# One wait for each TensorE instruction, and new places of the attention items' steps, in a fused attention and two-layer feed-forward kernel

## The chip, the cores and the metric

One NeuronCore of a Trainium2 chip runs the whole program. The metric is the device time of one execution in microseconds, the median of three runs. The engines are called TensorE (PE, with PEld for its weight loads), VectorE (DVE), ScalarE (ACT), GpSimd (POOL) and SyncE (SP).

## The reference

```python
# attention: q, k, v are (4, 8, 576, 64)
scores = scale * np.matmul(q, k.transpose(0, 1, 3, 2))
mask = block_i >= block_j                       # blocks of 64 positions
scores = np.where(mask, scores, -1000000000.0)
scores = scores - np.max(scores, axis=-1, keepdims=True)
attn = np.exp(scores)
attn = attn / (np.sum(attn, axis=-1, keepdims=True) + 1e-09)
out = np.matmul(attn, v)                        # -> x, (2304, 512)
# first layer
h = x @ w_in                                    # (2304, 2048)
g = np.where(h >= 1, h, np.where(h <= -1, 0.0, (h + 1) ** 2 / 4))
x = g @ w_out                                   # (2304, 512)
# second layer
h = x @ w_in2
g = h * np.cos(h)
return g @ w_out2
```

## The kernel before

**Precision.** Each operand of a product is split into a rounded part (`_hi`) and a remainder (`_lo`). A product of two is made of three matmuls (hi by hi, hi by lo, lo by hi), or of two where the two halves are stacked. So nearly every tensor is made twice: a copy on ScalarE (`x_hi`, `k_hi`, `q_hi`, `v_hi`, `pt_hi`, `g_hi`, `win_hi`, `wout_hi`), and a subtraction on VectorE (`x_lo`, `q_lo`, `pt_lo`, `win_lo`) or GpSimd (`k_lo`, `v_lo`, `g_lo`, `wout_lo`).

**Items.** Attention is cut into 64 items. The first 32, the early ones, are a head's first 256 queries (two tiles of 128), and the last 32, the late ones, are a head's other 320 queries (tiles of 128, 128 and 64). An item goes through these steps: scores on TensorE (`score`, L984), the row maximum on VectorE, the exponential with its row sums on ScalarE, the inverse of the sums on VectorE, the normalisation on GpSimd (`norm`), the transposes on TensorE (`turn`, L1008, into PSUM banks `turned` or `heads_out`), their split (`pt_hi` on ScalarE, `pt_lo` on VectorE), the weighing of V on TensorE (`weigh`, L1024, into `heads_out`), the move of one half of the result on ScalarE, and its addition on VectorE, which writes the feed-forward layer's input. The first and the third tile's transposes of a late item share the bank `turned`: the third tile's (`turn(n, 2)`) wait until `pt_lo` has read the first's.

**Stages.** Nine items run alone (0 to about 65 us), two beside each other in their own banks. The other 55 run beside the first layer's first seven tiles of 256 tokens (to about 540 us). Then come the first layer's last two tiles and the second layer's nine (from about 645 us), eight of them in a loop that the hardware runs. A tile of a layer is eight pairs of hidden blocks: `make_hidden` (L1076) fills a PSUM bank, the other engines activate it, and `use_hidden` (L1095) multiplies the result into `acc`, two pairs later. After a tile ScalarE reads `acc` out (`y_stage`, L696) and splits the next tile's input (`split_next_x`, L689).

**What sets the order.** Every engine runs its instructions in the order in which its own block of the program issues them. The items' steps are spread over slots: an item takes 11 slots (early) or 19 (late), and the table `AT` says at which slot of the item each step is issued, one number for each of three kinds of item: alone, early beside the layer, late. All engines walk the same slots, and within one slot the order of the `if`s in their `attention` function decides. Beside the layer `slots_beside` puts about two slots beside each half of a unit; a half is six matmuls of `make_hidden` or `use_hidden`. A late item so lasts about 10.5 us. `SPLIT_AT` and `LOAD_AFTER` say at which place the first layer's weight pieces are split (`win` on ScalarE and VectorE, `wout` on ScalarE and GpSimd) and after which item they are loaded.

**Waits.** Every step waits for counting semaphores of the steps it needs. On TensorE several waits stand directly ahead of one matmul, for instance ahead of both score matmuls:

```python
pe.wait_ge(q_lo_made, n + 1)
pe.wait_ge(k_lo_made, n + 1)
if late(n):
    pe.wait_ge(exp_made, first_tile(n) + (2 if i == 4 else 0))
```

Of the kernel before, what the change touches and what calls it, by code (L numbers as in the profile page):

```python
# [22 lines left out]
KC = DM // P  # L23
# [3 lines left out]
LAG = 2  # L27
# [42 lines left out]
def stat(n, i):  # L70
# [11 lines left out]
    "score": (0, 0, 0), "score_c": (0, 0, 7), "turn": (14, 12, 11), "turn_b": (0, 0, 16),  # L82
    "turn_c": (0, 0, 19), "weigh": (18, 18, 21), "k_hi": (-9, -9, -10), "q_hi": (-9, -8, -11),
    "v_hi": (8, 9, 6), "exp": (6, 3, 0), "exp_b": (6, 3, 2), "exp_c": (0, 0, 8),
    "pt_hi": (14, 11, 10), "pt_hi_b": (0, 0, 12), "pt_hi_c": (0, 0, 15), "move": (19, 16, 21),
    "q_lo": (-6, -7, -8), "max": (1, 0, 0), "max_b": (1, 0, 2), "max_c": (0, 0, 7),
    "inv": (5, 4, 2), "inv_b": (6, 4, 6), "inv_c": (0, 0, 11), "pt_lo": (14, 12, 15),
    "pt_lo_b": (0, 0, 17), "pt_lo_c": (0, 0, 19), "add": (19, 18, 23), "k_lo": (-9, -10, -11),
    "norm": (3, 3, 3), "norm_b": (6, 3, 5), "norm_c": (0, 0, 8), "x_hi": (20, 0, 0),
    "x_lo": (21, -3, -8), "begin": (20, -3, -6), "v_lo": (14, 7, 6),  # L90
# [20 lines left out]
def user_before(n):  # L111

    return n - 2 if n < ALONE else n - 1

# [30 lines left out]
SPLIT_AT = ((1, 3, 5, 9, 12, 17, 20, 24), (7, 10, 16, 18, 22, 26, 30, 35))  # L145
LOAD_AFTER = ((-1, 1, 4, 7, 9, 11, 12, 14), (-1, 8, 10, 12, 13, 15, 16, 17))
# [32 lines left out]
def attention_feed_forward(nc, qk_early, qk_late, v_early, v_late, w1_in, w1_out, w2_in, w2_out, x2_dram, out):  # L179
    with ExitStack() as ctx:  # L180
# [801 lines left out]
        def _(pe):  # L982
            def score(n, i):
                e = i - tiles_of(n)[0]  # L984
                pe.wait_ge(q_lo_made, n + 1)
                pe.wait_ge(k_lo_made, n + 1)

                if late(n):
                    pe.wait_ge(exp_made, first_tile(n) + (2 if i == 4 else 0))
                elif n > ALONE:  # L990
                    pe.wait_ge(exp_made, first_tile(n - 1) + e + 1)
                elif n > 1:
                    pe.wait_ge(exp_made, first_tile(n - 1 if n < ALONE else n))
# [6 lines left out]
                for into, first, end in pieces:  # L1000
                    nc.tensor.matmul(into, q_tile, k_hi_of(n)[:, first:end], start=True, stop=False)  # L1001
                    last = nc.tensor.matmul(into, q_tile, k_lo_of(n)[:, first:end], start=False, stop=True)  # L1002
                last.then_inc(scores_made, 1)

            def turn(n, e):
# [8 lines left out]
                elif user_before(n) >= 0:  # L1014
                    pe.wait_ge(pt_lo_made, first_turn(user_before(n) + 1))
# [177 lines left out]
```

## Time and profile before

| | |
|---|---|
| median of 3 runs | 1045.59 us (1045.02 to 1050.85) |
| the profiled execution | 1051.79 us |
| its span, first to last instruction | 1049.6 us |
| mean granted TensorE clock over the span | 0.981 |
| busy: TensorE, its weight loads | 1001.9 us (95%), 943.1 us (90%) |
| busy: VectorE, ScalarE, GpSimd | 657.0 (63%), 590.8 (56%), 426.5 us (41%) |
| matmuls | 7360 |

The profile is of one execution, and its durations belong to that one. A matmul's duration is modelled and overlaps the next one's, so how fast TensorE goes is read from the distances between starts, and short waits do not show as idle time of PE. Its weight load precedes each matmul; a wait that a matmul carries holds this load.

### The profile page before, as it was taken

How to read it: one execution, taken by the hardware profiler on the slowest of the kernel's cores; microseconds unless marked ns; L12 is line 12 of the kernel's file. 1: busy time of each engine (PE TensorE's matmuls, PEld its weight loads, DVE VectorE, ACT ScalarE, POOL GpSimd, SP SyncE). 2: the span in 40 equal slices, each digit the busy share in tenths (PEclk: the TensorE clock that was granted, in tenths of full speed). 3: DMA queues.
4: the chain of work that ended last, by engine and by line, in shares of the span. 5: the costliest groups of instructions: out<-in, count | busy, mean ns of one | idle time of the engine just before them, and what ended most of it. 6: DMA issues, size and time to landing. Idle time of an engine off the chain costs nothing.

```text
span 1049.6 us, 19879 instructions
## 1 busy us (share of the span) xinstructions
PE 1001.9 (95%) x7360; PEld 943.1 (90%) x7360; DVE 657.0 (63%) x1422; ACT 590.8 (56%) x1232; POOL 426.5 (41%) x446
## 2 busy tenths in 40 slices
PE   4688999999999999999999999999999999999997
PEld 3578999999999999999999998999999999999995
DVE  5567777766766767666732378656565555656553
ACT  5567776766666666666633356544444444445442
POOL 3559765555555554655522221222222222222211
PEclk9579999999999999999999999999999999999999
DMA  4335321221211212121200144010110101001000
GB/s 133 104 118 157 98 90 65 72 70 49 92 49 53 89 49 72 70 72 65 69 31 22 41 161 162 1 40 0 40 40 0 40 0 40 21 19 40 0 21 21
DMA packets 30886, 62.28 MB, mean 59 GB/s; under 512 B 3680, under 2 KB 11872, under 8 KB 30816
## 3 DMA queue, kind: packets, MB, share of 16 engines
q1 hardware_dynamic: 29664, 57.16, 17.1%
q10 hardware_dynamic: 1152, 4.19, 1.1%
q8 instruction: 43, 0.70, 0.3%
q14 instruction: 27, 0.22, 0.1%
HBM read 51.90 MB, written 9.44 MB: 58 GB/s over the span
## 4 chain that ended last, share of the span: by engine, by line
PE 79%; DVE 9%; ACT 5%; issue 3%; POOL 1%; DMA 1%; ACTq 0%; POOLq 0%; DVEq 0%
PE hidden L1090 33%; PE acc L1107 18%; PE acc L1115 12%; PE heads_out L1036 4%; PE scores L1001 4%; PE turned L1019 3%; PE scores L1002 3%; DVE neg_max L800 1%; PE heads_out L1019 1%; DVE x_lo L879 1%; PE hidden L1073 1%; DVE wout_lo L865 1%; DVE work L885 1%; ACT probs L616 1%; DVE pt_lo L817 1%
## 5 line engine op out<-in xcount | busy, mean ns | idle before, releaser
L543 POOL TENSOR_TENSOR g_lo<-work,g_hi 128x512 fp32r<-128x512 f32 x144 | 187.9, 1305 | 450.7 <-ACT g_hi L713 450.7
L1090 PE MATMUL hidden<-x_hi,win_hi 128*128 128x256 f32 x1136 | 323.5, 285 | 2.8 <-DVE work L912 1.2
L1090 PE MATMUL hidden<-x_hi,win_lo 128*128 128x256 f32 x1136 | 317.9, 280 | 0.0
L1090 PE MATMUL hidden<-x_lo,win_hi 128*128 128x256 f32 x1136 | 317.9, 280 | 0.0
L1090 PEld LDWEIGHTS hidden<-x_hi,win_hi 128*128 128x128 f32 x1136 | 214.3, 189 | 7.6 <-issue 2.0
L1090 PEld LDWEIGHTS hidden<-x_lo,win_hi 128*128 128x128 f32 x1136 | 214.2, 189 | 3.3
L1090 PEld LDWEIGHTS hidden<-x_hi,win_lo 128*128 128x128 f32 x1136 | 216.4, 190 | 0.0
L1115 PE MATMUL acc<-g_hi,wout_hi 128*128 128x256 f32 x576 | 167.4, 291 | 0.3 <-ACT y_stage L696 0.3
L1115 PE MATMUL acc<-g_lo,wout_hi 128*128 128x256 f32 x576 | 160.6, 279 | 0.0
L1115 PE MATMUL acc<-g_hi,wout_lo 128*128 128x256 f32 x576 | 160.5, 279 | 0.0
L513 POOL TENSOR_SCALAR probs<-probs,row_inv 64x576 f32<-64x576 f32 (+2 forms) x160 | 107.4, 675 | 121.6 <-DVE row_inv L812 120.8
L723 ACT ACTIVATE work<-work 128x512 f32<-128x512 f32 x72 | 45.5, 632 | 140.3 <-DVE work L902 140.3
L616 ACT ACTIVATE probs<-scores,neg_max 64x576 f32<-64x576 f32 (+2 forms) x160 | 90.5, 567 | 58.6 <-DVE neg_max L800 56.5
L1107 PE MATMUL acc<-wout_hi,g_hi 128*128 128x512 f32 x288 | 113.7, 395 | 1.6 <-POOL g_lo L543 1.6
L1107 PE MATMUL acc<-wout_hi,g_lo 128*128 128x512 f32 x288 | 113.4, 394 | 0.0
L1107 PE MATMUL acc<-wout_lo,g_hi 128*128 128x512 f32 x288 | 112.6, 391 | 0.0
L1115 PEld LDWEIGHTS acc<-g_hi,wout_hi 128*128 128x128 f32 x576 | 108.9, 189 | 1.2 <-issue 0.4
L1115 PEld LDWEIGHTS acc<-g_lo,wout_hi 128*128 128x128 f32 x576 | 109.2, 190 | 0.6
L912 DVE TENSOR_TENSOR work<-hidden,work 128x512 f32<-128x512 f32 x72 | 49.8, 692 | 94.9 <-ACT work L725 94.9
L1115 PEld LDWEIGHTS acc<-g_hi,wout_lo 128*128 128x128 f32 x576 | 108.9, 189 | 0.0
L713 ACT ACTIVATE g_hi<-work 128x512 fp32r<-128x512 f32 x144 | 89.8, 624 | 14.7 <-DVE work L890 12.3
L800 DVE TENSOR_REDUCE neg_max<-scores 64x1 f32<-64x576 f32 (+2 forms) x160 | 86.8, 543 | 17.7 <-PE scores L1002 13.1
(91 smaller groups left out, 1830.1 us busy)
## 6 DMA issues: line engine op xcount, KB each, us to landing
qk_raw<-qk_late SPq DMA_DIRECT2D x32, 448.0 KB, 3.2
qk_raw<-qk_early SPq DMA_DIRECT2D x32, 256.0 KB, 2.6
v_raw<-v_late SPq DMA_DIRECT2D x32, 160.0 KB, 3.3
x_raw<-x_scratch SPq DMA_DIRECT2D x9, 512.0 KB, 3.5
out<-y_stage SPq DMA_DIRECT2D x36, 128.0 KB, 2.4
x_raw<-w_in SPq DMA_DIRECT2D x8, 512.0 KB, 3.6
y_stage<-w_out SPq DMA_DIRECT2D x8, 512.0 KB, 3.5
x_scratch<-y_stage ACTq DMA_DIRECT2D x8, 512.0 KB, 2.7
```

The costliest lines, as they stand in the source:

```text
L513: nc.gpsimd.tensor_scalar(tile, tile, row_inv[0:rows_of(i), col:col + 1], 1.0, ALU.mult, ALU.mult).then_inc(probs_made, 1)
L543: nc.gpsimd.tensor_tensor(g_lo[:, m % G_RING, :], work[:, m % 2, :], g_hi[:, m % G_RING, :], ALU.subtract).then_inc(g_lo_made, 1)
L616: nc.scalar.activation(tile, scores_tile(n, i), ACT.Exp, bias=neg_max[0:rows_of(i), col:col + 1], accum_out=row_sum[0:rows_of(i), col:col ...
L713: nc.scalar.activation(g_hi[:, m % G_RING, :], work[:, m % 2, :], ACT.Copy).then_inc(g_hi_made, 1)
L723: nc.scalar.activation(work[:, m % 2, :], work[:, m % 2, :], ACT.Abs).then_inc(angle_abs, 1)
L800: nc.vector.tensor_reduce(out=neg_max[0:rows_of(i), col:col + 1], in_=scores_tile(n, i), axis=AX_XY if i == 4 else AX_X, op=ALU.max, negat ...
L912: nc.vector.tensor_tensor(work[:, m % 2, :], hidden[:, m % 2, :], work[:, m % 2, :], ALU.mult).then_inc(hidden_read, 1)
L1001: nc.tensor.matmul(into, q_tile, k_hi_of(n)[:, first:end], start=True, stop=False)
L1019: last = nc.tensor.transpose(turned_of(n, e)[:, at:at + q], probs_chunk(n, i, j), ident[0:q, 0:q])
L1090: last = nc.tensor.matmul(into, w[:, p, c, half * P:(half + 1) * P], x[:, c, :], start=(i == 0), stop=(i == len(products) - 1))
L1107: last = nc.tensor.matmul(acc[:, a, :], g[:, slot, at:at + P], w[:, p, half, :], start=(p == 0 and half == 0 and i == 0), stop=(end and i ...
L1115: last = nc.tensor.matmul(into, w[:, p, half, d * P:(d + 1) * P], g[:, slot, half * TOK:(half + 1) * TOK], start=(p == 0 and half == 0 and ...
```

## The change

It does three things. TensorE's waits are spread so that almost every instruction carries one: a wait that another one implies is left out, the scores' wait for `k_lo` goes to the second matmul, and waits that can be met earlier are put ahead of an earlier matmul (`steps_ahead`, `hidden_ahead`, `use_ahead`). The table `AT` has new places, among them the transposes (`turn`), the weighing (`weigh`), the splits of k, q and v, and the last tile's inverse (`inv_c`). Some weight splits and loads move by a place.

```diff
-    "score": (0, 0, 0), "score_c": (0, 0, 7), "turn": (14, 12, 11), "turn_b": (0, 0, 16),
-    "turn_c": (0, 0, 19), "weigh": (18, 18, 21), "k_hi": (-9, -9, -10), "q_hi": (-9, -8, -11),
...
+    "score": (0, 0, 0), "score_c": (0, 0, 7), "turn": (17, 12, 13), "turn_b": (0, 0, 16),
+    "turn_c": (0, 0, 19), "weigh": (19, 19, 21), "k_hi": (-11, -10, -11), "q_hi": (-11, -8, -11),
...
-SPLIT_AT = ((1, 3, 5, 9, 12, 17, 20, 24), (7, 10, 16, 18, 22, 26, 30, 35))
-LOAD_AFTER = ((-1, 1, 4, 7, 9, 11, 12, 14), (-1, 8, 10, 12, 13, 15, 16, 17))
+SPLIT_AT = ((1, 3, 5, 9, 12, 17, 20, 24), (7, 9, 16, 18, 21, 26, 30, 34))
+LOAD_AFTER = ((-1, 1, 3, 7, 9, 10, 12, 14), (-1, 8, 10, 12, 13, 15, 16, 18))
...
+def banks_seen(n):
+
+    before = n - 2 if n < ALONE else n - 1
+    last = "inv_c" if late(before) else "inv_b"
+    return n < 2 or slot_of(last, before) - sum(slots_of(m) for m in range(before, n)) <= slot_of("q_lo", n)
...
             def score(n, i):
                 e = i - tiles_of(n)[0]
-                pe.wait_ge(q_lo_made, n + 1)
-                pe.wait_ge(k_lo_made, n + 1)
-
-                if late(n):
-                    pe.wait_ge(exp_made, first_tile(n) + (2 if i == 4 else 0))
-                elif n > ALONE:
-                    pe.wait_ge(exp_made, first_tile(n - 1) + e + 1)
-                elif n > 1:
-                    pe.wait_ge(exp_made, first_tile(n - 1 if n < ALONE else n))
+
+
+                if e == 0:
+                    pe.wait_ge(q_lo_made, n + 1)
+                    if not banks_seen(n):
+                        pe.wait_ge(exp_made, first_tile(n))
+                elif e == 2:
+                    pe.wait_ge(exp_made, first_tile(n) + 2)
...
                     nc.tensor.matmul(into, q_tile, k_hi_of(n)[:, first:end], start=True, stop=False)
+                    if e == 0:
+                        pe.wait_ge(k_lo_made, n + 1)
...
             def turn(n, e):
...
                 pe.wait_ge(probs_made, first_tile(n) + e + len(tiles))
-
-                if e == 1:
-                    pe.wait_ge(heads_read, n)
-                elif e == 2:
-                    pe.wait_ge(pt_lo_made, first_turn(n) + 1)
-                elif user_before(n) >= 0:
-                    pe.wait_ge(pt_lo_made, first_turn(user_before(n) + 1))
...
+            def steps_ahead(n, k):
+
+                for m, j in near(n, k):
+                    if kind(m) == 1 and j == slot_of("weigh", m):
+                        pe.wait_ge(v_lo_made, m + 1)
+                    if late(m) and j == slot_of("turn_b", m):
+                        pe.wait_ge(heads_read, m)
+                    if late(m) and j == slot_of("turn_c", m):
+                        pe.wait_ge(pt_lo_made, first_turn(m) + 1)
+
             def weigh(n):
+
+
+
                 pe.wait_ge(pt_lo_made, first_turn(n) + (3 if late(n) else 1))
-                pe.wait_ge(v_lo_made, n + 1)
-                if user_before(n) >= 0:
-                    pe.wait_ge(heads_read, user_before(n) + 1)
+                if kind(n) == 0:
+                    pe.wait_ge(v_lo_made, n + 1)
...
+            def hidden_ahead(t, m):
+
+
+                pe.wait_ge(hidden_read, PAIRS * t + m + 1)
+
+            def use_ahead(t, p, first):
+
+                if p == 0:
+                    pe.wait_ge(g_lo_made, PAIRS * t + p + 1 + 2)
+                elif first:
+                    pe.wait_ge(wout_lo_made, p + 1)
...
-                if half == 0:
-                    pe.wait_ge(hidden_read, PAIRS * t + m + 1)
...
+                    if i == len(products) // 2 - 1:
+                        ahead_of_half(beside, 2 * u)
...
+                    if i == len(products) - 2 and ahead is not None:
+                        ahead()
+                    if i == len(products) - 1:
+                        ahead_of_half(beside, 2 * u + 1)
```

How this moves instructions, at four places. The lines on the left are those of each version's own text; the brackets are the semaphores that an instruction waits for.

TensorE where a late item ends and the next begins: the transposes of the last tile (64 columns) and the next item's first scores. Before:

```order
1334 L1115 MATMUL acc<-g_hi,wout_lo 128x256
1335 L1019 MATMUL turned<-ident,probs 128x64 [waits pt_lo_made,probs_made]
1336 L1019 MATMUL turned<-ident,probs 128x64 x4
1337 L1001 MATMUL scores<-k_hi,q_parts 128x384 [waits exp_made,k_lo_made,q_lo_made]
1338 L1002 MATMUL scores<-k_lo,q_parts 128x384
1339 L1001 MATMUL scores<-k_hi,q_parts 128x512 [waits exp_made,k_lo_made,q_lo_made]
```

And now:

```order
1334 L1160 MATMUL acc<-g_hi,wout_lo 128x256 [waits pt_lo_made]
1335 L1023 MATMUL turned<-ident,probs 128x64 [waits probs_made]
1336 L1023 MATMUL turned<-ident,probs 128x64 x4
1337 L1007 MATMUL scores<-k_hi,q_parts 128x384 [waits q_lo_made]
1338 L1010 MATMUL scores<-k_lo,q_parts 128x384 [waits k_lo_made]
1339 L1007 MATMUL scores<-k_hi,q_parts 128x512
```

No instruction moved here; the waits did. The first tile's transposes (three of 128 columns, at slot 13 and no longer 11) are issued six matmuls later in nearly all late items.

TensorE in an early item beside the first layer, around the weighing of V (`heads_out`). Before:

```order
202 L1090 MATMUL hidden<-x_hi,win_lo 128x256
203 L1036 MATMUL heads_out<-pt_hi,v_parts 128x256 [waits heads_read,v_lo_made,pt_lo_made]
204 L1036 MATMUL heads_out<-pt_lo,v_parts 128x256
205 L1036 MATMUL heads_out<-pt_hi,v_parts 128x128
206 L1036 MATMUL heads_out<-pt_lo,v_parts 128x128
```

And now:

```order
202 L1127 MATMUL hidden<-x_hi,win_lo 128x256
203 L1127 MATMUL hidden<-x_hi,win_hi 128x256
...
208 L1127 MATMUL hidden<-x_hi,win_lo 128x256 [waits v_lo_made]
209 L1052 MATMUL heads_out<-pt_hi,v_parts 128x256 [waits pt_lo_made]
210 L1052 MATMUL heads_out<-pt_lo,v_parts 128x256
```

The weighing stands six matmuls later.

ScalarE in a late item where the next tile's input is split (`x_hi`). Before:

```order
356 L616 ACTIVATE probs,row_sum<-scores,neg_max 64x576 [waits turned_made,max_made]
357 L602 ACTIVATE q_parts<-qk_raw 128x320 [waits scores_made,qk_in_0]
358 L689 ACTIVATE x_hi<-x_raw 128x512 [waits heads_read,hidden_made]
359 L689 ACTIVATE x_hi<-x_raw 128x512
360 L595 ACTIVATE k_hi<-qk_raw 128x576 [waits scores_made,qk_in_0]
361 L625 ACTIVATE pt_hi<-turned 128x3x128 [waits heads_made,turned_made]
```

And now:

```order
356 L623 ACTIVATE probs,row_sum<-scores,neg_max 64x576 [waits turned_made,max_made]
357 L602 ACTIVATE k_hi<-qk_raw 128x576 [waits scores_made,qk_in_0]
358 L609 ACTIVATE q_parts<-qk_raw 128x320 [waits scores_made,qk_in_0]
359 L696 ACTIVATE x_hi<-x_raw 128x512 [waits heads_read,hidden_made]
360 L696 ACTIVATE x_hi<-x_raw 128x512
361 L632 ACTIVATE pt_hi<-turned 128x3x128 [waits heads_made,turned_made]
```

`k_hi` went ahead of `q_hi` (the write of `q_parts`) and of the two `x_hi`.

ScalarE in a late item where a tile's result is read out (`y_stage`). Before:

```order
384 L602 ACTIVATE q_parts<-qk_raw 128x320 [waits scores_made,qk_in_0]
385 L595 ACTIVATE k_hi<-qk_raw 128x576 [waits scores_made,qk_in_0]
386 L696 ACTIVATE y_stage<-acc 128x1024 [waits y_stored,g_used]
387 L699 DMA x_scratch<-y_stage 128x1024 [waits acc_read]
388 L625 ACTIVATE pt_hi<-turned 128x3x128 [waits heads_made,turned_made]
```

And now:

```order
385 L609 ACTIVATE q_parts<-qk_raw 128x320 [waits scores_made,qk_in_0]
386 L632 ACTIVATE pt_hi<-turned 128x3x128 [waits heads_made,turned_made]
387 L703 ACTIVATE y_stage<-acc 128x1024 [waits y_stored,g_used]
388 L706 DMA x_scratch<-y_stage 128x1024 [waits acc_read]
389 L632 ACTIVATE pt_hi<-heads_out 128x4x128 [waits turned_made]
```

`y_stage` went behind `pt_hi` of the first tile. On VectorE `pt_lo` of the first tile went ahead of a clamp or a product of the layer in about half of the late items.

## Rows read from the trace of the kernel before

**Rows 1.** Stages: stretch, its length, each engine's busy time, clock, DMA share, GB/s.
```profile
0.00:65.00 65.00, 38.00 (x162) 32.76 (x163) 36.33 (x120) 34.49 (x97) 28.08 (x46) 0.74 0.36 116
...
100.00:190.00 90.00, 88.14 (x746) 86.72 (x747) 69.32 (x218) 64.10 (x185) 59.35 (x84) 1.00 0.28 90
190.00:535.00 345.00, 339.01 (x2722) 326.55 (x2721) 237.27 (x623) 224.16 (x502) 192.68 (x197) 1.00 0.20 65
```
**Rows 2.** Waits of TensorE's weight loads, 190 to 535 us: total, times, longest.
```profile
PEld scores L1001 <- issue: 3.7, 6, 1.0
PEld turned L1019 <- issue: 3.0, 6, 0.9
PEld turned L1019 <- POOL probs L513: 0.9, 2, 0.6
```
**Rows 3.** The same, 100 to 190 us, then 65 to 100 us.
```profile
PEld heads_out L1036 <- DVE pt_lo L817: 1.9, 4, 0.9
...
PEld heads_out L1036 <- DVE pt_lo L817: 3.1, 2, 2.4
```
**Rows 4.** Timeline, scores of a third tile without a late wait: start, duration.
```profile
235.25 0.28 PE L1090 MATMUL hidden<-x_hi,win_lo 128*128 128x256 f32 x1
235.37 0.29 PE L1001 MATMUL scores<-k_hi,q_parts 128*128 128x288 f32 x1
```
**Rows 5.** Timeline, the same step behind a late exponential.
```profile
299.98 0.19 ACT L616 ACTIVATION_READ_ACCUMULATOR probs<-scores,neg_max 128x1 f32 x1
...
300.09 0.28 PE L1090 MATMUL hidden<-x_hi,win_lo 128*128 128x256 f32 x1
...
300.32 0.37 PE L1001 MATMUL scores<-k_hi,q_parts 128*128 128x288 f32 x1
```
**Rows 6.** Timeline, from the split of x to a late item's first scores.
```profile
248.36 1.14 ACT L689 ACTIVATE x_hi<-x_raw 128x512 fp32r<-128x512 f32 x2
...
250.65 1.03 POOL L513 TENSOR_SCALAR probs<-probs,row_inv 64x576 f32<-64x576 f32 x1 [2.60 <-DVE row_inv L812]
...
251.65 1.40 POOL L506 TENSOR_TENSOR k_lo<-qk_raw,k_hi 128x576 fp32r<-128x576 f32 x1
...
253.15 0.41 PE L1001 MATMUL scores<-k_hi,q_parts 128*128 128x384 f32 x1 [0.85 <-issue]
253.40 0.34 PE L1002 MATMUL scores<-k_lo,q_parts 128*128 128x384 f32 x1
```
**Rows 7.** Timeline, VectorE's weight split ahead of a late pt_lo.
```profile
81.26 1.82 DVE L858 TENSOR_TENSOR win_lo<-x_raw,win_hi 128x1024 fp32r<-128x1024 f32 x1 [1.53 <-ACT win_hi L668]
```
**Rows 8.** Timeline, two tiles' read-outs and what follows them on TensorE.
```profile
271.35 1.01 ACT L696 ACTIVATE y_stage<-acc 128x1024 f32<-128x1024 f32 x1
...
272.83 0.36 PE L1115 MATMUL acc<-g_hi,wout_hi 128*128 128x256 f32 x1
...
274.05 0.49 PE L1019 MATMUL turned<-ident,probs 64*128 64x64 f32 x5 [0.27 <-DVE pt_lo L817]
...
347.29 1.01 ACT L696 ACTIVATE y_stage<-acc 128x1024 f32<-128x1024 f32 x1
...
348.65 0.36 PE L1115 MATMUL acc<-g_hi,wout_hi 128*128 128x256 f32 x1
```
**Rows 9.** Timeline, the second layer's first hidden block that waits.
```profile
654.73 0.69 DVE L912 TENSOR_TENSOR work<-hidden,work 128x512 f32<-128x512 f32 x1 [1.45 <-ACT work L725]
...
655.48 0.39 PE L1090 MATMUL hidden<-x_hi,win_hi 128*128 128x256 f32 x1 [1.20 <-DVE work L912]
```
**Rows 10.** Timeline, transposes and their splits in a late item without a wait.
```profile
464.57 0.49 PE L1019 MATMUL turned<-ident,probs 128*128 128x128 f32 x3
...
465.84 0.47 ACT L625 ACTIVATE pt_hi<-turned 128x384 fp32r<-128x384 f32 x1
...
466.35 0.56 DVE L817 TENSOR_TENSOR pt_lo<-turned,pt_hi 128x384 fp32r<-128x384 f32 x1 [0.46 <-ACT pt_hi L625]
...
468.25 0.52 PE L1019 MATMUL turned<-ident,probs 64*128 64x64 f32 x5
```

More of the change, by code:

```diff
@@ L81 @@
 AT = {
-    "score": (0, 0, 0), "score_c": (0, 0, 7), "turn": (14, 12, 11), "turn_b": (0, 0, 16),
-    "turn_c": (0, 0, 19), "weigh": (18, 18, 21), "k_hi": (-9, -9, -10), "q_hi": (-9, -8, -11),
[L84 to L90, printed above, removed]
+    "score": (0, 0, 0), "score_c": (0, 0, 7), "turn": (17, 12, 13), "turn_b": (0, 0, 16),
+    "turn_c": (0, 0, 19), "weigh": (19, 19, 21), "k_hi": (-11, -10, -11), "q_hi": (-11, -8, -11),
+    "v_hi": (11, 9, 6), "exp": (6, 3, 0), "exp_b": (8, 3, 2), "exp_c": (0, 0, 8),
+    "pt_hi": (13, 10, 9), "pt_hi_b": (0, 0, 13), "pt_hi_c": (0, 0, 15), "move": (20, 16, 21),
+    "q_lo": (-6, -7, -7), "max": (1, 0, 0), "max_b": (1, 0, 2), "max_c": (0, 0, 7),
+    "inv": (5, 4, 2), "inv_b": (8, 4, 6), "inv_c": (0, 0, 9), "pt_lo": (14, 12, 13),
+    "pt_lo_b": (0, 0, 17), "pt_lo_c": (0, 0, 19), "add": (21, 20, 23), "k_lo": (-9, -10, -11),
+    "norm": (6, 3, 1), "norm_b": (7, 3, 4), "norm_c": (0, 0, 8), "x_hi": (20, -5, 1),
+    "x_lo": (21, -4, -3), "begin": (20, 0, -6), "v_lo": (12, 7, 4),
 }
@@ L1063, in beside_half, with ahead_of_half @@
                         attention(n, k)
+            def ahead_of_half(beside, half):
+                if beside:
+                    for n, k in beside[half]:
+                        steps_ahead(n, k)
             def begin_hidden(c):
@@ L1093, in make_hidden, with use_hidden @@
                     last.then_inc(hidden_made, 1)
-            def use_hidden(t, p, half, second, beside=None, u=0):
-                if half == 0:
+            def use_hidden(t, p, half, second, beside=None, u=0, ahead=None):
+                if half == 0 and p == 0:
+                    pe.wait_ge(acc_read, t + 1)
+                elif half == 0:
                     pe.wait_ge(g_lo_made, PAIRS * t + p + 1 + 2)
-                    if p == 0:
-                        pe.wait_ge(acc_read, t + 1)
                 slot = p % G_RING
@@ L1105, in use_hidden @@
                         for i, (w, g) in enumerate(parts):
+                            if a == 1 and i == 1 and ahead is not None:
+                                ahead()
                             at = half * TOK + a * P
@@ L1113, in use_hidden @@
                         for i, (w, g) in enumerate(parts):
+                            if d == KC // 2 - 1 and i == 2:
+                                ahead_of_half(beside, 2 * u)
+                            if d == KC - 1 and i == 1 and ahead is not None:
+                                ahead()
+                            if d == KC - 1 and i == 2:
+                                ahead_of_half(beside, 2 * u + 1)
                             into = acc[:, d // 2, (d % 2) * TOK:(d % 2 + 1) * TOK]
@@ L1155, in _ @@
                     attention(n, k)
+            hidden_ahead(0, LAG)
             for t in range(BESIDE_TILES):
```

42 lines of the change are left out of this document (24 added, 18 removed).

## The prediction

> **What bounds the kernel now.** I read the stages first, then who waited for whom on TensorE's weight loads in each stage, then the timeline at each kind of wait.
>
> The stages [rows 1]: from 190 to 535 us TensorE is busy for 339.0 of 345 us, while VectorE, ScalarE and GpSimd are at 69%, 65% and 56%. The rest of TensorE's time there is work it cannot shed, so only microseconds in which it stands still can be won. In the first 65 us it is busy for 38.0 us at a mean granted clock of 0.74: there the heads are computed alone, and a chain through all engines sets the time.
>
> How much stands still, by the idle time of the weight loads (a modelled matmul end hides short gaps, a weight load's does not): from 190 to 535 us, 3.7 us ahead of the scores, 3.0 and 0.9 us ahead of the transposes [rows 2], and 0.8 us elsewhere; from 100 to 190 us, 1.9 us ahead of the weighing of V, and from 65 to 100 us, 3.1 us [rows 3]. That is about 13 us, plus many short gaps below the view's limit. These 13 us are what all of the change's new places can win behind the first 65 us.
>
> **The change part by part.**
>
> *One wait per matmul.* The listing of the program's waits has 393 TensorE instructions with two or more waits before and 19 after. What does such an instruction cost? Where all its semaphores had come early, nothing: the scores of the third tile at 235.37 carry three waits and start 0.12 us behind the matmul ahead of them, the step of any two 256-column matmuls [rows 4]. Where the last one is late, it costs. At 300.32 the exponential's sum, the release, ends at 299.98 + 0.19 = 300.17, and the matmul starts 0.15 us later and 0.23 us behind the one before it [rows 5]. A single wait that is late costs 0.05 us from release to start: the second layer's first late hidden block, at 655.48, starts 0.06 us behind the product that ends at 654.73 + 0.69 = 655.42 [rows 9]. So a late extra wait is 0.10 us dearer. The step of rows 5 stands 18 times among the 32 late items (the others step as in rows 4): 18 x 0.10 = **-1.8 us**; it cannot exceed 18 x 0.12 = 2.2 us, nor be less than 0 if the release itself moves.
>
> The Trainium skill says of this (Perfetto Trace Analysis, Identifying Dependency Chains) that an instruction which waits on several engines may have a separate semaphore instruction put ahead of it. If each of those cost TensorE the 0.11 us by which rows 5 exceed rows 4, all the removed ones would give some 40 us; rows 4 speak against it, so the sum goes by the late ones alone.
>
> *k_lo is waited for at the second matmul.* The scores of a late item wait 0.85 us at 253.15, because GpSimd has the normalisation of the last tile (250.65, 1.03 us) ahead of k_lo (251.65 to 253.05) [rows 6]. The new wait lets the first matmul go, 0.25 us (253.15 to 253.40), and drops the extra 0.10 us. Some four waits in the 3.7 us of rows 2 are of this kind (the rest are of rows 5's kind): 4 x 0.3 = **-1.2 us**, bounds 0 and -2.5. The new place of k_hi ahead of q_hi on ScalarE helps less than it looks, since the normalisation still stands ahead of k_lo on GpSimd.
>
> *That k_hi now stands ahead of x_hi in one item.* At 248.36 the two splits of x_hi come first; the two x_lo behind them on VectorE, in order ahead of the last tile's row sums, keep these back, thus the normalisation at 250.65, and thus TensorE [rows 6]. In the new order k_hi (0.57 us from start to start) is ahead of x_hi, so this chain ends that much later: **+0.6 us**, bounds 0 and 0.7.
>
> *The weighing of V, six matmuls later in the early items beside the first layer.* Six matmuls at the step of rows 4 are 6 x 0.12 = 0.7 us of cover. In the 1.9 us of rows 3 (four waits, the longest 0.9) that leaves 0.2: **-1.7 us**. Of the two waits between 65 and 100 us, the short one of 0.7 goes. The other is the one of 2.4 us: VectorE does win_lo from 81.26 for 1.82 us, then the row maxima, then pt_lo [rows 7]. ScalarE's win_hi, for which win_lo waits, now stands behind pt_hi, and so is 0.6 us later; the six matmuls give that back. Together **-0.8 us**. Bounds of the three: 0 and -3.7 (0.7 in each of the six waits at most, less what hides). What was queued behind the weighing: ScalarE's move of its result stands in order ahead of the next exponentials; in the early items ScalarE has 26 us idle in these 90 us, so I charge nothing, and at most 0.1 us for each of 23 items.
>
> *Transposes, two slots later; pt_lo ahead of the clamp on VectorE.* The transposes of an item's last tile need the bank that pt_lo of its first tile frees. At 274.05 they waited 0.27 us because y_stage (271.35, 1.01 us) stood ahead of pt_hi on ScalarE [rows 8]; the new order turns these two round: **-0.35 us**, with the extra wait. The other transposes' waits come from a late exponential or from the x splits, whose order stays. I take 0 for them; the bounds are +1 and -3.5.
>
> *y_stage behind pt_hi or behind k_hi.* In the item of rows 8 y_stage now starts about 0.5 us later; its end was 272.36, and the accumulators are next written at 272.83, so 0.2 us shows. In the tile at 347.29 it ends at 348.30 and the accumulators are written at 348.65 [rows 8]; k_hi (0.6 us) goes ahead of it, and 0.3 us shows. **+0.5 us**, bounds 0 and 1.
>
> *Waits put one or two matmuls ahead.* Where such a wait is late, the matmuls between it and the one that needs it no longer run in its shadow. At the first tile of the second layer [rows 9] these are two of 512 columns, each twice the 0.12 us step of 256: **+0.5 us**. Elsewhere in the second layer I expect nothing: since the products that end there have their activation done well before, and only this first tile shows such a late wait.
>
> *Weight splits moved by a place, GpSimd's v_lo ahead of k_lo, win_hi ahead of v_hi in the first 65 us.* These go into idle time of ScalarE and GpSimd (30 and 37 us idle of 65 [rows 1]), and the order of TensorE's own instructions is the same there: 0, bounds -1 and +1.
>
> Sum: -1.8 - 1.2 + 0.6 - 1.7 - 0.8 - 0.35 + 0.5 + 0.5 = **-4.25 us**. The profiled execution took 1051.79 us (span 1049.6), and would take 1047.5. It is 6.2 us above the median of the three runs, 1045.59; the terms do not depend on that, so the median should come to 1041.3 us.
>
> **The rivals.**
>
> *Nothing is won.* Each place that is late is late by a chain of three engines. Freed at one point, the wait appears at the next: the transposes of the last tile behind the scores, the accumulators behind y_stage. For: two of my eight terms are already such returns. Against: the 18 steps of rows 5 end in a dearer form of wait and not in a queue. Time: 1045.6, give or take 1.
>
> *The new places do more than I can follow.* Every wait listed from 65 to 535 us goes (13 us) and the late extra waits with them (1.8), less 1 us of the returns: 1045.6 - 13.8 = 1032. Against: VectorE's x_lo and GpSimd's normalisation keep their order in the two longest of them.
>
> *All extra semaphore instructions cost.* 0.11 us for each of some 390: 1003 us. Rows 4 say no.
>
> *Slower: the transposes are moved past the point of no slack.* The first tile's transposes start 0.7 us later in nearly all late items. In an item with no wait pt_lo ends at 466.35 + 0.56 = 466.91 and the last tile's transposes start at 468.25: 1.34 us of slack [rows 10]. In the items where VectorE has the clamp or the product (0.69 us) ahead of pt_lo, some 0.7 is left, and the new wait is one matmul earlier (0.11). If pt_hi followed its transposes directly, the later start would pass on in full, and each wait of ScalarE behind it too: 0.4 us in each of 32 items is +12.8, and with the other terms +8.5: 1054. It decides from the point at which pt_lo ends within 0.2 us of the transposes. For: the slack is the smallest of any in the item. Against: pt_hi starts at 465.84 in rows 10, 1.27 us behind the transposes' start at 464.57, straight after k_hi; so ScalarE's queue, and not the transposes, sets it.
>
> **How the numbers follow.** Chances: forecast 0.58, nothing won 0.22, more than followed 0.09, all extras 0.02, slower 0.09. The forecast's own spread from the terms' bounds is -9 to +1.5 us. The range from 1033 to 1049 us leaves out the case of all extras, the better half of the larger gain and the slower case. A measurement of this kernel can tell about 1% (10 us) from no change. Faster by that needs a time below 1035.1: most of the larger gain, the case of all extras and a tail of the forecast, 0.15. Slower by that needs more than 1056: a part of the slower case and some unforeseen loss of clock in the first 90 us, 0.05. The rest, 0.80, is within 1%.
>
> **What would show it.** Right: the scores of the third tile step by 0.11 to 0.14 us in all late items; the weighing of V between 100 and 190 us waits less than 0.5 us in all; the scores at the first x split of the late items still wait. Wrong: new waits of the last tile's transposes on pt_lo in most items (the slower rival); an idle total of the weight loads from 190 to 535 us below 2 us (the larger gain); or a first stage whose length or granted clock differs, which none of my terms contains.

## The result, and the profile after

The changed kernel takes 1087.28 us (median of 4 runs, 1084.63 to 1094.19), the kernel before 1045.3 us. The ratio is 1.040, its 95% interval 1.034 to 1.046: 42 us slower, where I had forecast 4 us faster. The four executions of the changed kernel lie 10 us apart, so the loss is known as 35 to 48 us.

The profiled execution took 1085.11 us. The page of the changed kernel, the span and the busy times (share of the span, instructions):

```profile
span 1082.9 us, 19481 instructions
PE 1007.5 (93%) x7360; PEld 944.1 (87%) x7360; DVE 702.5 (65%) x1422; ACT 590.1 (54%) x1232; POOL 417.1 (39%) x446
```

TensorE's work did not grow: its weight loads are busy for 944.1 us against 943.1. VectorE has the same 1422 instructions and is busy for 45.5 us more (657.0 before). That number names the engine, and it is what to follow.

The waits of TensorE's weight loads from 190 to 580 us, which answer to [rows 2] (the late items now last until about 580 us):

```profile
PEld acc L1160 <- DVE pt_lo L824: 24.2, 21, 3.3
PEld hidden L1127 <- DVE pt_lo L824: 13.6, 10, 2.4
PEld scores L1007 <- ACT probs L623: 1.4, 2, 1.1
PEld scores L1010 <- POOL k_lo L513: 0.9, 2, 0.5
PEld heads_out L1052 <- DVE pt_lo L824: 0.7, 2, 0.4
PEld acc L1160 <- ACT y_stage L703: 0.6, 2, 0.3
```

The first two rows are one wait: the one for `pt_lo` of an item's first tile that `steps_ahead` puts one matmul ahead of the last tile's transposes. It stands 31 times, once for each late item but one, and takes 37.8 us. The scores' waits of [rows 2] did shrink: six of 3.7 us in all there, four of 2.3 us here (1.4 on the exponential, 0.9 on `k_lo`).

Why is `pt_lo` late? VectorE's groups by shape, before and then after. The columns behind the bar are busy time, mean ns of one, and idle time before:

```profile
L789 DVE SCALAR_TENSOR_TENSOR q_parts<-qk_raw,q_parts 64x320 fp32r<-64x320 f32 x32 | 16.8, 525 | 1.0
L817 DVE TENSOR_TENSOR pt_lo<-turned,pt_hi 128x384 fp32r<-128x384 f32 x60 | 33.3, 555 | 15.1 <-ACT pt_hi L625 14.4
```
```profile
L796 DVE SCALAR_TENSOR_TENSOR q_parts<-qk_raw,q_parts 64x320 fp32r<-64x320 f32 x32 | 65.9, 2060 | 8.4 <-ACT q_parts L609 7.8
L824 DVE TENSOR_TENSOR pt_lo<-turned,pt_hi 128x384 fp32r<-128x384 f32 x60 | 33.4, 556 | 5.1 <-ACT pt_hi L632 3.6
```

`pt_lo` is as long as ever. `q_lo` (the write of `q_parts` from `qk_raw` and `q_parts`), the same instruction on the same 64 x 320 numbers, takes 2060 ns instead of 525: 32 x 1.535 = 49.1 us more. One late item of the changed kernel, in the timeline:

```profile
462.25 0.15 DVE L819 RECIPROCAL row_inv<-row_sum 64x1 f32<-64x1 f32 x1
462.33 0.69 DVE L892 TENSOR_SCALAR work<-hidden 128x512 f32<-128x512 f32 x1
462.50 0.75 POOL L520 TENSOR_SCALAR probs<-probs,row_inv 64x576 f32<-64x576 f32 x1
462.52 0.46 ACT L609 ACTIVATE q_parts<-qk_raw 128x320 fp32r<-128x320 f32 x1
462.88 0.49 ACT L632 ACTIVATE pt_hi<-turned 128x384 fp32r<-128x384 f32 x1
463.06 1.94 DVE L796 SCALAR_TENSOR_TENSOR q_parts<-qk_raw,q_parts 64x320 fp32r<-64x320 f32 x1
463.22 1.43 POOL L513 TENSOR_TENSOR k_lo<-qk_raw,k_hi 128x576 fp32r<-128x576 f32 x1
...
465.03 0.56 DVE L824 TENSOR_TENSOR pt_lo<-turned,pt_hi 128x384 fp32r<-128x384 f32 x1
...
465.64 0.39 PE L1160 MATMUL acc<-g_hi,wout_lo 128*128 128x256 f32 x1 [0.38 <-DVE pt_lo L824]
```

And the same place in the kernel before (the item of [rows 10]):

```profile
465.22 0.15 DVE L812 RECIPROCAL row_inv<-row_sum 64x1 f32<-64x1 f32 x1
...
465.40 0.49 DVE L789 SCALAR_TENSOR_TENSOR q_parts<-qk_raw,q_parts 64x320 fp32r<-64x320 f32 x1
465.47 1.04 POOL L513 TENSOR_SCALAR probs<-probs,row_inv 64x576 f32<-64x576 f32 x1 [0.44 <-DVE row_inv L812]
...
466.49 1.41 POOL L506 TENSOR_TENSOR k_lo<-qk_raw,k_hi 128x576 fp32r<-128x576 f32 x1
```

Read the ends. Before, `q_lo` starts 0.07 us ahead of GpSimd's normalisation; `q_lo` takes 0.49 us, and the normalisation 1.04. After, the normalisation starts 0.56 us ahead; it takes 0.75 us, `k_lo` follows without a gap, and `q_lo` ends at 465.00, 0.35 us behind the end of `k_lo` (463.22 + 1.43 = 464.65). So one of the two engines stands still for most of the time in which the other runs, and the profile books that as busy time of the one that stands. A search for idle time does not find it.

The Trainium skill describes this (SBUF — State Buffer, Who interferes with whom): VectorE and GpSimd share a pair of ports into SBUF under an exclusive lock, which a VectorE instruction with two inputs in SBUF needs against a GpSimd instruction that reads SBUF; the first holds it for its whole length. `q_lo` has two such inputs; `pt_lo` has one in PSUM, and kept its 556 ns.

Three of the change's entries bring `q_lo` behind the normalisation, and each of them looked harmless by itself. `k_hi` ahead of `q_hi` on ScalarE makes `q_hi`, for which `q_lo` waits, 0.57 us later. `inv_c` at slot 9 instead of 11 releases the normalisation earlier. `q_lo` at slot -7 instead of -8 stands later. By the last two, a clamp or a product stands between the reciprocal and `q_lo` in 16 of 31 late items; before, in none.

The waits on `pt_lo` are not the whole loss. From 100 us to its last few microseconds the kernel before has a granted clock of 1.00 throughout. The changed kernel has 0.50, the lower of the two levels (1.2 and 2.4 GHz), for 3.4 us at three places, and 1.00 again behind each. The first three lines are these places, the last is the stretch behind the third:

```profile
199.80:203.10 3.30, 3.30 (x13) 3.10 (x13) 2.96 (x9) 1.62 (x4) 0.00 (x0) 0.50 0.43 163
261.20:264.60 3.40, 3.40 (x17) 3.40 (x16) 1.35 (x5) 0.67 (x2) 0.86 (x2) 0.50 0.61 186
428.50:431.80 3.30, 3.30 (x15) 2.99 (x15) 1.99 (x6) 1.11 (x3) 0.00 (x0) 0.50 0.54 183
432.00:435.30 3.30, 3.30 (x28) 3.24 (x27) 1.05 (x6) 1.57 (x4) 0.74 (x2) 1.00 0.00 0
```

TensorE does 13 to 17 matmuls in such a stretch and 28 in the same time at 1.00. My estimate from these rows is 1.5 us lost at each, some 5 us in all. Within the 2.5 us before each, a wait of TensorE on `pt_lo` had ended: of 1.4, 1.2 and 3.0 us. One of 3.3 us, at 515 us, is followed by no such stretch, so the length of one wait does not decide it.

### The profile page after: what moved, and what is told of

Its sections match the earlier page's. It is cut to its first block, busy times and chain, and to the rows that moved or that the text cites. A ratio compares the mean times of both kernels' runs of the same rounds, so it can differ in the third digit from the quotient of the medians.

```text
span 1082.9 us, 19481 instructions
## 1 busy us (share of the span) xinstructions
PE 1007.5 (93%) x7360; PEld 944.1 (87%) x7360; DVE 702.5 (65%) x1422; ACT 590.1 (54%) x1232; POOL 417.1 (39%) x446
## 4 chain that ended last, share of the span: by engine, by line
PE 68%; DVE 17%; ACT 7%; issue 6%; POOL 1%; DMA 1%; ACTq 0%; POOLq 0%; DVEq 0%
PE hidden L1127 28%; PE acc L1146 17%; PE acc L1160 8%; DVE q_parts L796 5%; PE heads_out L1052 5%; PE scores L1007 3%; PE scores L1010 2%; DVE pt_lo L824 2%; DVE neg_max L807 2%; PE turned L1023 2%; DVE work L892 2%; ACT probs L623 1%; DVE wout_lo L872 1%; DVE work L897 1%; ACT k_hi L602 1%
## 5 line engine op out<-in xcount | busy, mean ns | idle before, releaser
L1127 PEld LDWEIGHTS hidden<-x_hi,win_lo 128*128 128x128 f32 x1136 | 213.9, 188 | 14.9 <-DVE pt_lo L824 13.6
L1160 PE MATMUL acc<-g_hi,wout_lo 128*128 128x256 f32 x576 | 163.5, 284 | 20.7 <-DVE pt_lo L824 20.0
L520 POOL TENSOR_SCALAR probs<-probs,row_inv 64x576 f32<-64x576 f32 (+2 forms) x160 | 98.5, 619 | 169.6 <-DVE row_inv L819 168.9
```

What stands on the lines that cost most here:

```text
L520: nc.gpsimd.tensor_scalar(tile, tile, row_inv[0:rows_of(i), col:col + 1], 1.0, ALU.mult, ALU.mult).then_inc(probs_made, 1)
L1127: last = nc.tensor.matmul(into, w[:, p, c, half * P:(half + 1) * P], x[:, c, :], start=(i == 0), stop=(i == len(products) - 1))
L1160: last = nc.tensor.matmul(into, w[:, p, half, d * P:(d + 1) * P], g[:, slot, half * TOK:(half + 1) * TOK], start=(p == 0 and half == 0 and ...
```

## The experiments

Theory A: `q_lo`, started behind the normalisation, is held by GpSimd, and `pt_lo` behind it in VectorE's order holds TensorE. Rival B: the spread waits cost. Rival C: the transposes, two slots later, have no slack left (my slower rival). Rivals D and E stand with the runs that tell them apart. A late item "is held" when its `q_lo` takes over 0.9 us in the profile; 31 late items are counted, all but the first, which follows an early one. Each ratio is against executions of the kernel before that were timed together with that run.

**The spread waits alone** (the changed kernel with `AT`, `SPLIT_AT` and `LOAD_AFTER` of before):

> The spread waits of the change with the tables of before. Theory A (VectorE's q_lo is held up by GpSimd because the tables move it behind the start of the last normalisation): q_lo of the late items stays at about 0.5 us, no long waits of TensorE on pt_lo, 1 to 4 us faster than before (about 1043). Rival B (the bank's wait for pt_lo, put one matmul earlier and on its own, is what costs): about 1085. Rival C (the transposes two slots later leave no slack): about 1043 as A.

Measured: 1043.05 us, ratio 0.9988 (0.9979 to 0.9998). No item is held, the 32 `q_lo` take 532 ns on average. B falls. The spread waits are worth about 1.3 us, just clear of the noise.

**The new tables alone** (the kernel before with the three tables of the change):

> The new tables with the waits of before. Theory A: q_lo takes about 1.9 to 3.2 us in about 29 of 32 late items, the last tile's transposes wait 30 to 37 us in all for pt_lo, time 1083 to 1090. Rival B (the waits cost): about 1045. Rival C (transposes too late): 1083 to 1090 as A.

Measured: 1082.87 us, ratio 1.0393 (1.0356 to 1.0429); 29 of 31 items are held, and the last tile's transposes wait for 33.6 us. The time is 0.1 us under the range of A and C. The whole loss is in the tables. A and C both stand.

**q_hi ahead of k_hi again**, in the changed kernel:

```diff
-                    if j == slot_of("k_hi", m):
+                    if not late(m) and j == slot_of("k_hi", m):
                         split_k_hi(m)
                     if j == slot_of("q_hi", m):
                         split_q_hi(m)
+                    if late(m) and j == slot_of("k_hi", m):
+                        split_k_hi(m)
```

> The changed kernel, with q_hi ahead of k_hi on ScalarE in the late items, nothing else. Theory A: in the 15 or so late items in which q_lo follows the reciprocal directly it now starts before the normalisation and takes 0.5 us; in the other 16, with a clamp or product between, it still takes about 1.9 us. Time 1065 to 1072. Rivals B and C: 1085, and q_lo's duration decides nothing.

Measured: 1061.5 us, ratio 1.0166 (1.0149 to 1.0183); 16 items are held, as counted from the order. The waits on `pt_lo`:

```profile
PEld acc L1162 <- DVE pt_lo L826: 11.5, 14, 1.9
PEld hidden L1129 <- DVE pt_lo L826: 6.7, 7, 1.3
```

The mechanism is as A has it. The time is 3.5 us below A's range: against the next run (1044.2) the 16 items that are still held cost 1.1 us each.

**Three places taken back** in the changed kernel (this edit, `"inv_c": (0, 0, 11)` and `"q_lo": (-6, -7, -8)`), with the transposes at their new slot 13:

> The changed kernel with three places taken back: q_hi ahead of k_hi on ScalarE, q_lo at slot -8 and inv_c at slot 11 again in the late items, so that q_lo directly follows the last reciprocal as before. The transposes stay at slot 13 and all waits stay spread. Theory A: q_lo takes 0.5 to 0.8 us in all items, the waits of 37 us go, time 1040 to 1048. Rivals B and C: 1080 or more.

Measured: 1044.21 us, ratio 1.0001 (0.9991 to 1.001); no item is held, and 3.7 us are left of the waits on `pt_lo`. C falls: the transposes' new place, with all the other new places that are left, costs at most the 1.2 us that lie between this run and the one with the spread waits alone.

**k_hi ahead of q_hi in the kernel before** (`"k_hi": (-9, -9, -11)`), one number:

> The kernel before, with one edit: k_hi ahead of q_hi on ScalarE in the late items. Theory A (q_lo loses its turn against GpSimd when it starts behind the last normalisation): q_hi ends 0.57 us later, q_lo starts after the normalisation and takes 1.9 us or more in nearly all late items; time 1072 to 1085, though the transposes stand where they stood. Rival C (the transposes' two slots are needed for the loss): under 1055.

Measured: 1096.56 us, ratio 1.0485 (1.0467 to 1.0502); 29 items are held, and the transposes wait for 44.9 us. One number makes this kernel slower than the whole change does. A had said 1072 to 1085, too little. Its trace shows two reasons. `pt_lo` here still stands at slot 15: in 18 of 31 items a clamp or a product lies between `q_lo` and it, and it starts 0.64 or 0.75 us behind the end of `q_lo`. In the run with the new tables alone that is so in 3 items, and its waits are 11.3 us shorter. And the granted clock is at 0.50 for 24 us between 190 and 600 us, where the new tables alone have 14. Neither was tried by itself.

**The last inverse two slots earlier in the kernel before**, again one number (`"inv_c": (0, 0, 9)`):

> The kernel before with one number changed: the inverse of the last tile's row sums at slot 9 instead of 11, thus earlier. In 12 of 31 late items a clamp or a product of VectorE now stands between that inverse and q_lo, and the normalisation starts before q_lo. Theory A: q_lo takes 1.9 us or more in these 12 and 0.5 to 0.8 in the others, 0.9 to 1.4 us lost for each: 1055 to 1062. If only the order of k_hi and q_hi mattered: 1045.

Measured: 1057.3 us, ratio 1.0118 (1.0101 to 1.0135); `q_lo` is held in 12 items and short in 19. TensorE's transposes wait (before: 3.0, 6, 0.9):

```profile
PEld turned L1019 <- issue: 17.4, 18, 1.6
```

A step that is done earlier makes the kernel slower, by 1.1 us for each held item.

**GpSimd only writes k_lo.** In the late items of the changed kernel k_lo is filled with zeros in the same place, so the low part of k is left out of these scores:

```diff
+                if late(n):
+                    nc.gpsimd.memset(k_lo_of(n)[:, 0:cols].bitcast(F32), 0.0).then_inc(k_lo_made, 1)
+                    return
                 nc.gpsimd.tensor_tensor(k_lo_of(n)[:, 0:cols], raw_k(n), k_hi_of(n)[:, 0:cols],
```

> The changed kernel, but GpSimd fills k_lo of the late items with zeros instead of subtracting: the same place and waits, an instruction that only writes, and the low part of k is left out of the scores. Theory A with the reads as the cause (q_lo has two operands in SBUF, GpSimd's subtraction and normalisation read SBUF): q_lo waits for the normalisation alone, 0.6 to 0.8 us instead of 1.9, TensorE's waits on pt_lo fall from 37 to under 8 us, time 1045 to 1055. Rival D (any GpSimd instruction beside it holds q_lo): q_lo lasts until the fill ends. Rival E (q_lo is long of itself at its new place): 1.9 us as before.

Measured: 1045.11 us, ratio 0.9986 (0.9962 to 1.001). One item in the timeline:

```profile
456.32 0.75 POOL L523 TENSOR_SCALAR probs<-probs,row_inv 64x576 f32<-64x576 f32 x1 [0.28 <-DVE row_inv L822]
456.84 0.57 DVE L799 SCALAR_TENSOR_TENSOR q_parts<-qk_raw,q_parts 64x320 fp32r<-64x320 f32 x1
457.01 0.58 POOL L514 MEMSET k_lo<- 128x576 f32 x1
457.43 0.56 DVE L827 TENSOR_TENSOR pt_lo<-turned,pt_hi 128x384 fp32r<-128x384 f32 x1
```

`q_lo` ends 0.34 us behind the end of the normalisation (457.07), while the fill runs until 457.59. So a GpSimd instruction that writes only does not hold it (D falls), and at its new place it is short as soon as nothing holds it (E falls). The same section of the Trainium skill says this: two inputs in SBUF contend with a GpSimd instruction that reads SBUF, not with one that only writes it.

**q_lo with one operand from SBUF.** In the late items of the changed kernel the subtraction of `q_hi` is left out:

```diff
+                if late(n):
+                    nc.vector.tensor_scalar(q_of(n)[D:2 * D, 0:cols], raw_q(n)[D:2 * D], SCALE, 1.0, ALU.mult,
+                                            ALU.mult).then_inc(q_lo_made, 1)
+                    return
```

> The changed kernel, but q_lo of the late items is a scaled copy of q with one operand from SBUF; the subtraction of q_hi is left out. Theory A with two operands as the cause: q_lo takes about 0.3 to 0.5 us at the same place and waits, though GpSimd runs beside it, time 1042 to 1050. Against it: if a one-operand form of it is held too, q_lo stays at 1.9 us and the time at 1085.

Measured: 1082.35 us (two executions), ratio 1.0353 (1.0332 to 1.0373); 29 items are held. A miss. Where nothing holds it, this form takes 0.32 us; beside GpSimd it is held as the other was:

```profile
459.84 1.78 DVE L797 TENSOR_SCALAR q_parts<-qk_raw 64x320 fp32r<-64x320 f32 x1
```

So two operands in SBUF are not the only case. A copy-like instruction from SBUF to SBUF is held too. The same section of the Trainium skill says so: a tensor_scalar can enter a mode that takes both port pairs. Instructions with an operand in PSUM were never held in these traces: `pt_lo`, the clamp (L892) and the product (L897) have the same duration beside GpSimd as without it. Nor were two short ones that stay in SBUF, the guard of the row sums and the reciprocal, with one number for each partition (0.13 to 0.17 us in all cases). So not every instruction from SBUF to SBUF is held.

**pt_lo ahead of q_lo** (the changed kernel with `"q_lo": (-6, -7, -5)`):

> The changed kernel with q_lo at slot -5 instead of -7 in the late items, thus behind pt_lo of the first tile on VectorE. Theory A: the loss comes from what is queued behind q_lo; pt_lo no longer waits for GpSimd, TensorE's waits on pt_lo of 37 us go for the most part. q_lo itself may still be held by k_lo, and the first scores wait for it at times. Time 1042 to 1056. Rival C (transposes too late): 1080 or more.

Measured: 1059.76 us, ratio 1.0128 (1.0108 to 1.0147), 4 us above the range. The waits on `pt_lo` went as A says, but 22 items are still held, mostly behind `k_lo` alone, and now the next scores wait for `q_lo` itself:

```profile
PEld scores L1007 <- DVE q_parts L796: 10.0, 10, 2.5
```

The granted clock is at 0.50 for 14 us between 190 and 560 us, an estimated 6 us more that my range did not have. To take the victim out of the queue moves the wait; it does not remove its cause.

**One wait more.** In the late items of the changed kernel, `k_lo` waits until `q_lo` is made:

```diff
+                if late(n):
+                    pool.wait_ge(q_lo_made, n + 1)
                 nc.gpsimd.tensor_tensor(k_lo_of(n)[:, 0:cols], raw_k(n), k_hi_of(n)[:, 0:cols],
```

> The changed kernel with one wait more: in the late items GpSimd's k_lo waits for VectorE's q_lo. All places stay as in the changed kernel. Theory A (q_lo gets no turn while GpSimd's reading instructions follow each other without a gap): q_lo gets in behind the normalisation and takes 0.5 to 0.85 us instead of 1.9, TensorE's waits on pt_lo fall from 37 to under 8 us, k_lo is 0.3 to 0.5 us later, and the time is 1043 to 1050 although a wait was added. If places or q_lo's own length decided: 1085 or more.

Measured: 1047.9 us, ratio 1.0034 (1.0023 to 1.0045): 39 us faster than the changed kernel by a wait that was added. The timeline:

```profile
458.71 0.74 POOL L522 TENSOR_SCALAR probs<-probs,row_inv 64x576 f32<-64x576 f32 x1 [0.28 <-DVE row_inv L821]
...
459.23 0.56 DVE L798 SCALAR_TENSOR_TENSOR q_parts<-qk_raw,q_parts 64x320 fp32r<-64x320 f32 x1
459.82 0.56 DVE L826 TENSOR_TENSOR pt_lo<-turned,pt_hi 128x384 fp32r<-128x384 f32 x1
459.94 1.42 POOL L515 TENSOR_TENSOR k_lo<-qk_raw,k_hi 128x576 fp32r<-128x576 f32 x1 [0.49 <-DVE q_parts L798]
```

GpSimd gives `q_lo` its turn and loses 0.49 us. TensorE's waits on `pt_lo` from 190 to 600 us fall to 4.5 us. The granted clock stays at 1.00 between 100 and 1040 us. What the wait costs is small: of the 3.4 us over the kernel before, about 1 us is TensorE's waits on `k_lo` between 0 and 600 us, which are 2.3 us here and 1.3 us with the spread waits alone:

```profile
PEld scores L1012 <- POOL k_lo L515: 2.3, 3, 1.4
```

By tiles, the difference stands in the first layer's third tile: 78.6 us here, 75.4 in the kernel before. TensorE's listed waits in it are 5.5 us against 2.8, among them one on `q_lo` of 1.1 us and one on `pt_lo` of 1.2 us.

**Is there a version that beats both?** The late column of the table as before, everything else as changed; and the same with `pt_lo` at slot 13:

> The changed kernel with the whole late column of the table as before; the new places of the alone and early items, the weight splits and the spread waits stay. Theory A: no long q_lo; the spread waits give 1.2 to 1.8 us (as alone), the weighing of V six matmuls later gives 1.6 us more between 120 and 180 us: 1040.5 to 1042.5. If the late column's other new places (transposes, pt_lo) had been worth something, it is slower than the kernel with three places taken back (1044.2).

> The same with pt_lo of the late items' first tile at slot 13, ahead of the clamp or the product on VectorE as in the changed kernel. The waits of the last tile's transposes on pt_lo (4.6 us in the run with the spread waits alone) fall to 2 to 3.5 us: 1039 to 1042, 0 to 2 us faster than the kernel without this edit.

Measured: 1044.79 us, ratio 0.9991 (0.9971 to 1.0012), and 1044.93 us, ratio 0.9989 (0.9969 to 1.0009). Both missed their ranges, and neither can be told from the kernel before. The weighing's 1.6 us are there: the first layer's second tile, from its first matmul to that of the third, lasts 60.4 us, against 61.9 with the spread waits alone. But the third tile lasts 76.2 us against 75.2, and most of it is given back. Which step gives it back is open. The only version whose interval lies below the kernel before is the one with the spread waits alone, by 0.1%.

## Why the prediction was wrong

**The sum left out q_lo.** The step that failed is the one on "that k_hi now stands ahead of x_hi in one item". I followed `k_hi` past `x_hi`, and did not follow what else it was moved past: `q_hi`, and with it `q_lo` on VectorE. The prediction names this order, for what it might win, and gives it no cost. The entries `q_lo` and `inv_c` have no term at all, and the transposes, where the loss shows, were put at 0 apart from one wait. In place of +0.6 us these three entries cost about 43 us: with them taken back, the time is 1044.2 instead of 1087.3. Of that, 34 us are TensorE's waits on `pt_lo` (37.8 against 3.7), and an estimated 5 us are the three stretches at the lower clock, of which the run without the three entries has none. The last few microseconds are not placed.

**The rule was in sight.** The kernel before shows it in its second layer, 70 times, where TensorE is busy throughout. VectorE's product of two tensors in SBUF lies in part beside `g_lo` and takes 1.17 us on average, where the two that were free of GpSimd took 0.69:

```profile
L902 DVE SCALAR_TENSOR_TENSOR work<-probs,work 128x512 f32<-128x512 f32 x72 | 84.3, 1171 | 2.5
```

The normalisation of 1.03 us in [rows 6] was the same sign: the changed kernel does it in 0.75. I took both for the instructions' own durations. Instructions of one form with two durations should have been asked which engine runs beside the long ones.

**The slower rival had the place, but not the mechanism.** It said that the last tile's transposes would wait for `pt_lo` of the first, and the trace shows just this wait, 31 times. It put it down to the transposes' later slot, at 0.4 us each; the run with three places taken back shows that this slot costs about 1 us at most in all, and the wait came from VectorE's queue at 1.2 us each. The slack of 1.34 us [rows 10] was read rightly, and so was the argument that ScalarE's queue sets `pt_hi`. A delay of 1.5 us in `q_lo` is what used this slack up.

**One wait per matmul, -1.8 us:** right in kind. In the changed kernel a late exponential is followed by the third tile's scores like this (it answers to [rows 5]):

```profile
216.88 0.19 ACT L623 ACTIVATION_READ_ACCUMULATOR probs<-scores,neg_max 128x1 f32 x1
216.99 0.28 PE L1127 MATMUL hidden<-x_hi,win_lo 128*128 128x256 f32 x1
...
217.13 0.40 PE L1007 MATMUL scores<-k_hi,q_parts 128*128 128x288 f32 x1
```

The release ends at 217.07, the matmul starts 0.06 us later and 0.14 us behind the one before; [rows 5] had 0.15 and 0.23. In all but two of the 32 late items this step is now 0.11 to 0.15 us, which was my first sign of being right. By [rows 9] a single late wait costs 0.06 us and not 0.05, so the term should have been -1.6. All that concerns the waits (-1.8, -1.2 and +0.5 in my sum, thus -2.5) measured -1.3 by itself. 374 instructions with several waits became one-wait instructions for that, so nearly all of them had cost nothing: the rival of 1003 us falls.

**k_lo at the second matmul, -1.2 us:** the scores' waits of [rows 2], on `k_lo` and on the exponential together, fell by 1.4 us (from six to four), and two of 0.9 us in all are still on `k_lo`. What the edit was worth alone was not measured. The edit also has a condition that I had not read off: the first matmul needs `k_hi` and no longer waits for `k_lo`, so `k_hi` has to stand ahead of something that is waited for. The order `k_hi`, `q_hi` gives that, but it isn't needed: the order of before has `k_hi` ahead of `pt_hi`.

**The weighing, -1.7 us beside the second tile:** right where it is (60.4 us for 61.9), and in the version with the late column of before most of it is given back one tile later. Between 100 and 190 us as a whole, the weighing still waits for 1.4 us; my sign had asked for less than 0.5. **The weighing from 65 to 100 us, -0.8 us:** its waits fell from 3.1 to 1.9 us, but waits on `v_lo` (2.1 us, of which 1.2 also with the spread waits alone) and on `q_lo` (1.3 us for 0.4) came in their place, and nothing was won.

**y_stage, +0.5 us:** 2 waits of 0.6 us in all, but one of them (0.4 us, at 197 us) stood in the kernel before too. Of the two new ones that I forecast, the one of 0.3 us is there and the one of 0.2 us is not.

**The first stage, 0:** the first layer's second tile starts at 118.3 us, at 118.6 before. That is luck in part. The mean granted clock from 0 to 65 us is 0.84 in the changed kernel and was 0.74, which I had named as a sign of being wrong. Three other runs have the changed kernel's early items and the clock of 0.74 (`k_lo` filled, `pt_lo` first, one wait more), and there this tile starts at 119.7 to 119.8 us. Why the clock differs is not known.

**The bounds.** The prediction gives the spread from the terms' bounds as -9 to +1.5 us. Added up, the bounds that it states give -12.4 to +4.2. The measured +42 lies outside both.

**The profiled execution of before.** It stands 6 us above its median, and that is no part of the change: of the 70 timed executions of the kernel before, 8 took 1050.3 to 1052.5 us and the other 62 at most 1046.4. (Four of them are among those that the two versions with the late column of before were compared with. They bring these ratios to 0.999, though by the medians, 1044.79 and 1044.93 against 1044.58 us, both are slower.) From 700 to 1000 us it does 1937 matmuls, the run with the spread waits alone 1971, at the same granted clock:

```profile
700.00:1000.00 300.00, 300.00 (x1937) 272.68 (x1936) 174.59 (x234) 144.98 (x229) 69.33 (x54) 1.00 0.08 21
```
```profile
700.00:1000.00 300.00, 300.00 (x1971) 273.39 (x1970) 177.81 (x239) 148.26 (x234) 69.90 (x54) 1.00 0.08 22
```

A second-layer tile lasts 44.75 us in the one and 43.95 us in all of the later profiles, among them those with the waits of before. Its cause is not known. It is the larger part of why the two spans differ by only 33 us where the medians differ by 42; the profiled execution of the changed kernel is also 2 us below its median.

## What to carry to other kernels

When a VectorE instruction whose tensors all lie in SBUF moves, ask which GpSimd instruction will then run beside it, and whether that one reads SBUF. If so, their order of start is part of the schedule, worth here 1.1 to 1.5 us of the kernel's time for each held item. An instruction whose mean duration differs between two kernels, or between two places of one kernel, may be a wait in disguise, and the profile page's busy times of the same number of instructions show it at once. Where two such instructions can't be kept apart by their places, a wait that makes GpSimd give way can pay for itself many times over.

## What was not expected of the hardware

A held VectorE instruction does not always get its turn between two GpSimd instructions that follow each other. In the late items the normalisation, `k_lo` and, where it came next, `g_lo` went through one after the other, and `q_lo` was held by three in a row and took up to 3.22 us. Where the normalisation came behind `v_lo` or `g_lo`, as in seven items of the kernel before, `q_lo` got in:

```profile
206.02 0.65 DVE L789 SCALAR_TENSOR_TENSOR q_parts<-qk_raw,q_parts 64x320 fp32r<-64x320 f32 x1
```
```profile
205.45 0.88 POOL L519 TENSOR_TENSOR v_parts<-v_raw,v_parts 128x320 fp32r<-128x320 f32 x1
206.31 0.99 POOL L513 TENSOR_SCALAR probs<-probs,row_inv 64x576 f32<-64x576 f32 x1
```

Here `v_lo` ends at 206.33, `q_lo` at 206.67, and this time the normalisation is the longer one. In the late items, what followed on GpSimd was a tensor_scalar, a fill, a wait or nothing wherever `q_lo` got in. But the kind of instruction does not decide it. In an early item of the kernel before, `q_lo` (64 x 256 numbers, 0.42 us when free) got in between two tensor_tensors:

```profile
95.12 2.41 POOL L537 TENSOR_TENSOR wout_lo<-y_stage,wout_hi 128x1024 fp32r<-128x1024 f32 x1
97.28 0.53 DVE L789 SCALAR_TENSOR_TENSOR q_parts<-qk_raw,q_parts 64x256 fp32r<-64x256 f32 x1
97.48 0.94 POOL L506 TENSOR_TENSOR k_lo<-qk_raw,k_hi 128x256 fp32r<-128x256 f32 x1
```

`wout_lo` ends at 97.53 and `q_lo` at 97.81, and `k_lo` takes 0.94 us where it takes 0.73 when free, though its `k_hi` had been ready since 96.07. What does decide it is open.
